# Block products with seven instead of eight multiplications in an attention and expert chain

## The reference, cut to what matters

```python
# 1. attention with decay, 2 x 8 heads, 768 tokens, head_dim 64, in blocks -> x [1536, 512]
# 2. experts
for e in range(4):                       # w1[e] 512 x 1024, w2[e] 1024 x 512
    h = np.maximum(x @ w1[e], 0.0)
    out += p[:, e:e + 1] * (h @ w2[e])
# 3. projection
a = x @ w1                               # 512 x 1024
b = x @ w2
h = a * b @ w3                           # 1024 x 1024
return h @ w_out                         # 1024 x 512
```

## Time and profile before

| | us |
|---|---|
| median of 3 runs | 829.05 (828.93 to 829.12) |
| the profiled execution | 828.76 |
| its span | 826.9 |
| PE busy | 819.8 |
| DVE, ACT, POOL busy | 272.7, 167.3, 153.8 |

### The profile page before, as it was taken

One profiled execution on the slowest core, in us unless ns is written; L12 is line 12 of the kernel. 1 busy time (PEld: TensorE's weight loads), 2 busy tenths in 40 slices (PEclk: granted clock), 3 DMA queues, 4 the chain that ended last, 5 costly groups with the idle time before them and its releaser, 6 DMA issues.

```text
span 826.9 us, 9271 instructions
## 1 busy us (share of the span) xinstructions
PE 819.8 (99%) x3994; PEld 670.5 (81%) x3994; DVE 272.7 (33%) x415; ACT 167.3 (20%) x281; POOL 153.8 (19%) x202
## 2 busy tenths in 40 slices
PE   9999999999999999999999999999999999999998
...
DMA packets 33544, 47.05 MB, mean 57 GB/s; under 512 B 3544, under 2 KB 13280, under 8 KB 33504
## 3 DMA queue, kind: packets, MB, share of 16 engines
...
...
## 4 chain that ended last, share of the span: by engine, by line
PE 97%; DVE 1%; issue 0%; POOL 0%; ACT 0%; POOLq 0%
PE banks L822 48%; PE banks L837 11%; PE banks L838 11%; PE banks L842 11%; PE banks L735 5%; PE banks L891 3%; PE banks L896 3%; PE banks L892 3%; PE banks L747 1%; PE banks L769 1%; PE banks L777 1%; PE banks L793 1%; PE banks L785 0%; DVE probs L599 0%; DVE fin L710 0%
## 5 line engine op out<-in xcount | busy, mean ns | idle before, releaser
L822 PE MATMUL banks<-xh,uph 128*128 128x512 f32 x480 | 189.6, 395 | 0.0
L822 PE MATMUL banks<-xh,upl 128*128 128x512 f32 x480 | 188.7, 393 | 0.0
L822 PE MATMUL banks<-xl,uph 128*128 128x512 f32 x480 | 187.1, 390 | 0.0
L478 ACT ACTIVATE hidh<-hid 128x512 fp32r<-128x512 f32 x120 | 75.9, 632 | 488.9 <-DVE hid L664 422.5
L664 DVE SCALAR_TENSOR_TENSOR hid<-banks,pb 128x512 f32<-128x512 f32 x96 | 66.3, 690 | 294.3 <-PE banks L822 294.3
L837 PE MATMUL banks<-hidh,dnh 128*128 128x512 f32 x384 | 151.1, 394 | 0.0
L838 PE MATMUL banks<-hidh,dnl 128*128 128x512 f32 x384 | 150.8, 393 | 0.0
L447 POOL TENSOR_TENSOR upl<-raw,uph 128x512 fp32r<-128x512 f32 x40 | 52.2, 1304 | 420.5 <-ACT uph L478 420.5
L558 DVE TENSOR_TENSOR hidl<-hid,hidh 128x512 fp32r<-128x512 f32 x120 | 83.5, 696 | 83.7 <-ACT hidh L478 83.7
L822 PEld LDWEIGHTS banks<-xh,upl 128*128 128x128 f32 x480 | 90.1, 188 | 21.5
L822 PEld LDWEIGHTS banks<-xl,uph 128*128 128x128 f32 x480 | 90.2, 188 | 20.9
...
## 6 DMA issues: line engine op xcount, KB each, us to landing
...
```

Source lines behind the costliest of these rows:

```text
L478: return nc.scalar.activation(dst, src, ACT.Copy)
L822: last = mm(bank, x, y, start=kt == 0 and i == 0, stop=kt == KT - 1 and i == 2)
```

## The change

The weights are taken by pairs of hidden tiles: FG = 4 pairs an expert. For token blocks 0 and 1 the product of a pair is seen as a product of 2 x 2 blocks: the weight's A11, A12, A21, A22 (tile by half of the 512 model columns), the tokens' B11, B12, B21, B22 (half of the model columns by token block). Seven block products, each KH = 2 pieces x 3 = 6 matmuls, replace eight: P1 = A11 B11, P2 = A12 B21, P3 = S4 B22, P4 = A22 T4, P5 = S1 T1, P6 = S2 T2, P7 = S3 T3. S and T are sums of blocks: T is made once per stage of tokens (by DVE, from `acc` before the experts and again before the projection), S for each pair (by POOL, `sums`). Token block 2 is multiplied as before (`third`, 12 matmuls a tile: Ua, Ub). One such unit of work is a run w; 16 serve the experts, 8 the projection (w1 and w2 in turn). The banks X, Y, Z are added to by several products, and DVE takes sums out on the way: v1 (by ACT, `snapshot`), u2, u3, c22, c21, c12.

The six hidden tiles of a run (two tiles by three blocks; ring, hh, hl) meet the second weights in the next run: 12 `group`s of 6 matmuls, each complete in one of five banks, and DVE adds each into `acc` (`add_group`), so the experts are summed in SBUF. For the experts the low part of a hidden tile is made by POOL (`hidden_low`), where DVE made it before. In the projection a first run (w1) leaves its six results in `a_tile`, the second (w2) multiplies by them and DVE makes the low parts.

Further: the folded matrix goes to DRAM and comes back a pair at a time like a weight; the attention's results of chunks 0 to 7 go through `acc` (ACT copies, then ACT and POOL split), those of chunks 8 to 11 are split at once as `xc`; the first two weight pairs are split during the fold, and none during the attention; chunk i is loaded to the place of chunk i - 6. The diff, cut to its core (lines taken out are left out, they stand in the functions printed above):

```diff
+                if 1 <= i <= ST:
+                    pool.wait_ge(b_hi, i)
+                    low(xs_l[:, B11:B21 + 1, :, tokens(i - 1)].rearrange("p b k n -> p (b k) n"),
+                        acc[:, :, tokens(i - 1)],
+                        xs_h[:, B11:B21 + 1, :, tokens(i - 1)].rearrange("p b k n -> p (b k) n")).then_inc(b_lo, 1)
+                if ST < i <= NB:
+                    pool.wait_ge(b_hi, i)
+                    low(xs_l[:, B22, :, tokens(i - 1 - ST)], acc[:, KH:KT, tokens(i - 1)],
+                        xs_h[:, B22, :, tokens(i - 1 - ST)]).then_inc(b_lo, 1)
...
+            def a_low(j):
+                s = j % 2
+                pool.wait_ge(wa_hi, j + 1)
+                low(w_l[s][:, A11:A22 + 1, :], up_src(j), w_h[s][:, A11:A22 + 1, :]).then_inc(wa_lo, 1)
+            def sums(j):
+                r = up_src(j)
+                pool.wait_ge(wa_lo, j + 1)
+                tt(r[:, A11, :], r[:, A11, :], r[:, A21, :], ALU.subtract).then_inc(ws_sum, 1)
+                pool.wait_ge(ws_sum, 4 * j + 1)
+                tt(r[:, A21, :], r[:, A21, :], r[:, A22, :], ALU.add).then_inc(ws_sum, 1)
+                pool.wait_ge(ws_sum, 4 * j + 2)
+                tt(r[:, A22, :], r[:, A22, :], r[:, A11, :], ALU.subtract).then_inc(ws_sum, 1)
+                pool.wait_ge(ws_sum, 4 * j + 3)
+                tt(r[:, A12, :], r[:, A12, :], r[:, A22, :], ALU.subtract).then_inc(ws_sum, 1)
...
+            for w in range(NQ):
+                later = 2 <= w + 1
+                if later:
+                    a_low(w + 1)
+                    sums(w + 1)
+                hidden_low(OUTS * w)
+                if later:
+                    s_low(w + 1)
+                hidden_low(OUTS * w + 1)
+                d_low(w)
+                for k in range(2, OUTS):
+                    hidden_low(OUTS * w + k)
...
+            def a_high(j):
+                if j < 2:
+                    act.wait_ge(up_first_ld[j], 16)
+                else:
+                    act.wait_ge(up_ld[j % 2], 16 * (j // 2))
+                    act.wait_ge(piece_done, made(j - 2, "Ub"))
+                copy(w_h[j % 2][:, A11:A22 + 1, :], up_src(j)).then_inc(wa_hi, 1)
+            def s_high(j):
+                act.wait_ge(ws_sum, 4 * (j + 1))
+                copy(w_h[j % 2][:, S3:S2 + 1, :], up_src(j)).then_inc(ws_hi, 1)
...
+                bank = out_bank(i).rearrange("p (a i) -> p a i", a=HP)
+                if i < NB:
+                    copy(acc[:, :, tokens(i)], bank).then_inc(att_left, 1)
+                    act.wait_ge(att_left, i + 1)
+                    if i == 0:
+                        act.wait_ge(fold_done, FT)
+                    if i < ST:
+                        copy(xs_h[:, B11:B21 + 1, :, tokens(i)].rearrange("p b k n -> p (b k) n"),
+                             acc[:, :, tokens(i)]).then_inc(b_hi, 1)
+                    else:
+                        copy(xs_h[:, B22, :, tokens(i - ST)], acc[:, KH:KT, tokens(i)]).then_inc(b_hi, 1)
+                else:
+                    copy(xc_h[:, :, tokens(i - NB)], bank).then_inc(xc_hi, 1)
+                    if i in (8, 9):
+                        t_high(0, i - 8)
+            for k in (2, 3):
+                t_high(0, k)
+            def snapshot(w):
+                act.wait_ge(piece_done, made(w, "P1"))
+                if w > 0:
+                    act.wait_ge(c21_ready, w)
+                copy(v1[:, :], bank_x).then_inc(v1_ready, 1)
+            def hidden_high(n):
+                Q, k = divmod(n, OUTS)
+                c = ORDER[k] // 2
+                act.wait_ge(r_ready, n + 1)
+                if Q > 0:
+                    act.wait_ge(group_done, GR * (Q - 1) + KT * (c + 1))
+                copy(hh[:, ORDER[k], :], ring_at(n)).then_inc(h_hi, 1)
+            for w in range(NQ):
+                later = 2 <= w + 1
+                snapshot(w)
+                if later:
+                    a_high(w + 1)
+                hidden_high(OUTS * w)
+                if later:
+                    s_high(w + 1)
+                hidden_high(OUTS * w + 1)
+                d_high(w)
+                for k in range(2, OUTS):
...
+            def t1_sum(phase):
+                tt(t1[:, :, :], x12, x11, ALU.subtract).then_inc(t_sum, 1)
+            def t2_sum(phase):
+                dve.wait_ge(b_lo, ST if phase == 0 else NB + KH)
+                dve.wait_ge(t_sum, 4 * phase + 1)
+                tt(x11, x22, t1[:, :, :], ALU.subtract).then_inc(t_sum, 1)
+            def t3_sum(phase):
+                tt(x12, x22, x12, ALU.subtract).then_inc(t_sum, 1)
+            def t4_sum(phase):
+                dve.wait_ge(b_lo, ST if phase == 0 else NB + 2 * KH)
+                dve.wait_ge(t_sum, 4 * phase + 2)
+                tt(x21, x21, x11, ALU.subtract).then_inc(t_sum, 1)
+            def t3_low(phase):
+                dve.wait_ge(t_hi, 4 * phase + 3)
+                sub(xs_l[:, T3, :, :], x12, xs_h[:, T3, :, :]).then_inc(t3_lo, 1)
             dve.wait_ge(state_zero, 1)
...
                 if n < NT - 1:
                     scale_q(i + 1)
...
+            def sum_u2(w):
+                dve.wait_ge(piece_done, made(w, "P6"))
+                dve.wait_ge(v1_ready, w + 1)
+                if w > 0:
+                    dve.wait_ge(c12_ready, w)
+                tt(u2[:, :], v1[:, :], bank_y, ALU.add).then_inc(u2_ready, 1)
+            def sum_u3(w):
+                dve.wait_ge(piece_done, made(w, "P7"))
+                if w > 0:
+                    dve.wait_ge(c22_ready, w)
+                tt(u3[:, :], v1[:, :], bank_y, ALU.add).then_inc(u3_ready, 1)
+            def sum_c22(w, dst):
+                dve.wait_ge(piece_done, made(w, "P5"))
+                dve.wait_ge(u3_ready, w + 1)
+                tt(dst, u3[:, :], bank_z, ALU.add).then_inc(c22_ready, 1)
+            def sum_c21(w, dst):
+                dve.wait_ge(piece_done, made(w, "P4"))
+                tt(dst, v1[:, :], bank_y, ALU.add).then_inc(c21_ready, 1)
+            def sum_c12(w, dst):
+                dve.wait_ge(piece_done, made(w, "P3"))
+                dve.wait_ge(u2_ready, w + 1)
+                tt(dst, u2[:, :], bank_z, ALU.add).then_inc(c12_ready, 1)
...
+            def gate(n, src):
+                j = ORDER[n % OUTS]
+                nc.vector.scalar_tensor_tensor(out=ring_at(n), in0=src, scalar=0.0, in1=pb[:, j // 2, :],
+                                               op0=ALU.max, op1=ALU.mult).then_inc(r_ready, 1)
+            def ring_free(n):
+                if n >= OUTS * NQ:
+                    dve.wait_ge(h_lo, n - 1)
+                elif n >= 3:
+                    dve.wait_ge(h_lo, n - 2)
+            def add_group(g):
+                Q, at = divmod(g, GR)
+                dve.wait_ge(group_done, g + 1)
+                if Q < NQ:
+                    c, d = divmod(at, KT)
                     cols = acc[:, d, c * CW:(c + 1) * CW]
...
+            for w in range(NQ):
+                e, q = divmod(w, FG)
+                n = OUTS * w
+                add_groups(w - 1, (0, 1))
+                sum_u2(w)
+                if w == 0:
+                    t3_low(0)
+                add_groups(w - 1, (2, 3, 4, 5))
+                if q == 0:
+                    for c in range(NC):
+                        dve.wait_ge(pb_ld[c], 16 * (e + 1))
+                dve.wait_ge(piece_done, made(w, "P2"))
+                ring_free(n)
+                gate(n, bank_x)
+                add_groups(w - 1, (6, 7))
+                sum_u3(w)
+                ring_free(n + 1)
+                sum_c22(w, ring_at(n + 1))
+                dve.wait_ge(c22_ready, w + 1)
+                gate(n + 1, ring_at(n + 1))
+                add_groups(w - 1, (8, 9, 10, 11))
+                dve.wait_ge(piece_done, made(w, "Ua"))
+                ring_free(n + 2)
+                gate(n + 2, bank_x)
+                ring_free(n + 3)
+                sum_c21(w, ring_at(n + 3))
+                dve.wait_ge(c21_ready, w + 1)
+                gate(n + 3, ring_at(n + 3))
+                ring_free(n + 4)
+                sum_c12(w, ring_at(n + 4))
+                dve.wait_ge(c12_ready, w + 1)
+                gate(n + 4, ring_at(n + 4))
+                dve.wait_ge(piece_done, made(w, "Ub"))
+                ring_free(n + 5)
+                gate(n + 5, bank_y)
...
+            def times(n, src, a):
+                tt(ring_at(n), src, a, ALU.mult).then_inc(r_ready, 1)
+            def hidden_low(n):
+                dve.wait_ge(h_hi, n + 1)
...
+                    sum_c21(w, a_tile[ORDER[3]])
+                    sum_c12(w, a_tile[ORDER[4]])
+                else:
+                    sum_u2(w)
+                    dve.wait_ge(piece_done, made(w, "P2"))
+                    dve.wait_ge(a_copied, 3 * (Q - NQ) + 1)
+                    ring_free(n)
+                    times(n, bank_x, a_tile[ORDER[0]])
+                    sum_u3(w)
+                    ring_free(n + 1)
```

(72 more changed lines are left out.)

907 lines of the change are left out of this document (488 added, 419 removed).

## The result

The changed kernel takes 804.89 us (median of 4 runs, 803.70 to 804.96), the kernel before beside it 829.02: a ratio of 0.971 (95% interval 0.969 to 0.972). The forecast was 800.0, with a range from 788 to 815. The profiled execution took 804.89 with a span of 803.1; before they were 828.76 and 826.9.

The account below looks back on a forecast made before the run. PE was taken as the bound, matmul count times 0.23 us plus the attention. 828.76 - 33.2 + 0.75 + 1.4 + 0.6 + 1.0 + 0.3 = 799.6, forecast 800 us, range 788 to 815.

Parts of the forecast that it names:

- The count: Expert and projection runs: 138 matmuls instead of 144 per run, 3216 wide ones instead of 3360, saving 33.2 us.
- The pace: Remaining matmuls keep the old 230.6 and 229.6 ns; at 227 ns 10 us more saved, equally far above costs 10.
- Rival (a): Clean pace: six matmuls on a bank without switching run like the fold, 227 ns, giving 790 us; chance 0.14.
- Order in the expert stage: Expert runs of 31.8 us without a stall; DVE 15.9, ACT 8.2, POOL 18.2 us hidden beside PE; tightest slack 0.5 us.
- (b): Boundary stalls: DVE is behind with an addition, each of 24 runs loses about 0.5 us, giving 812; chance 0.16.
- (c): POOL becomes the bound in expert runs through hidden low parts and SBUF shared with DVE, giving 845; chance 0.07.
- Attention and first run: Attention net +0.75 us from DVE slip less removed stalls; first run's waits at P2 and P7 +1.4, bounds 0 and 5.
- Into the projection: First projection run: the third block's low part, four DVE pieces behind u2, comes late for Ua: +0.6 us, bounds 0 and 3.
- the 1.8 us: Sign against the prediction: it is wrong if a low part of POOL takes over 1.8 us.
- Second runs of pairs: Projection: the sum freeing bank Y for Ub queues behind hidden_low; 0.35 us stall, four runs +1.0 us, bounds 0 to 3.
- End: The last twelve groups start on a low part that is 0.3 us late: +0.3 us; tail as before.
- the 227 to 234: Sign against the prediction: it is wrong if PE's pace leaves 227 to 234 ns.

Follow-up runs that it names:

- experiment 5: The changed kernel with block product P5 made twice into its bank, 144 matmuls more: 836.31 us, ratio 1.008 to the kernel before.
- experiment 9: The kernel before, each bank getting its three second-weight matmuls in a row (high by high, high by low, low by high): 828.97 or 829.13 us, ratio 1.000.
- experiment 10: The kernel before, one bank at a time in the second-weight product, but with the old matmul order inside a bank: 828.97 or 829.13 us, ratio 1.000.
- experiment 11: The kernel before as a bench: in ten stretches of the expert stage the second-weight product reads other operands, output not the reference: 825.90 us, one execution.
- experiment 12: The kernel before with only SBUF places changed: hidden tiles moved to the front of the late region, acc and fin behind them: 829.30 us, ratio 1.000.
- experiment 6: The changed kernel with sum c21 before hidden_low in second projection runs, and DVE making most low parts between stages while POOL stays off: 796.37 us, ratio 0.960.
- experiment 7: The 796.37 us version with ACT's copy of bank X moved ahead of the high parts of B22 and T4: 793.42 us, ratio 0.957.
- experiment 2: The changed kernel with POOL's low part of S in the projection made as four operations of 128x256 instead of one: 801.96 us, ratio 0.967.
- experiment 4: The changed kernel with POOL, into the projection, waiting until DVE has made the third block's four low parts: 804.54 us, ratio 0.971.
- experiment 1: The changed kernel with DVE's sum c21 ahead of the low part (hidden_low) in second runs of the projection: 801.98 us, ratio 0.967.
- experiment 8: The 793.42 us version with three changes of order: first-run snapshot earlier, u3 and T4's low part before B22's, last-run c21 after hidden_low: 792.66 us, ratio 0.956.

## Why the prediction was right or wrong

**The count** (-33.2) was right: 3216 wide matmuls, and experiment 5 shows their worth, 31.4 us for 144 with the waits that they cover.

**The pace** was mis-sized. I took 230.6 and 229.6 ns; the changed kernel runs at 226.7 throughout, 10.9 us less. Rival (a) had the size (10 us) and not the reason: it put the loss down to streams in which PE reads hidden tiles or changes banks. Experiments 9 and 10 show that the change of bank is not it. Experiment 11 shows that it is the tile that is read, but not because it is a hidden one: the route weights are as slow, and the groups of the changed kernel read hidden tiles at full pace. What it is about the tiles' place stays open (experiment 12). The fold's 227 ns, which I had as one end, was the pace of this kind of stream, and 230.6 belonged to the kernel before.

**Order in the expert stage** was right: no stall from the first groups to the last run of the experts, DVE 16.0 and POOL 18.2 us of 31.28. Rivals (b) and (c) fall. POOL's stretch is 1371 / 1304 = 1.05 on the hidden tiles. Most of DVE's operations there have an input in a bank and do not meet POOL.

**Attention and first run**: +0.75 became +1.3, +1.4 stayed +1.4, and +0.8 came on top: the first groups wait for POOL's low parts. In the first run, which has no groups, the hidden tiles come within 15 us; the low part of the second weights (2.40 us) goes ahead of the third of them, and two took 1.7 us instead of 1.3 beside DVE. Right in kind, each within its bounds.

**Into the projection** is the step that failed: 0.6 us, bounds 0 and 3, became 9.9 (2.8 at P6, 4.6 at Ua, 2.5 of slow clock). I named the right work, the third block's low parts ahead of Ua, and priced it at bare durations, 0.69 each. They took 1.8, and the double-width low part of T3 2.35 instead of the 1.2 it takes without POOL (experiments 6 and 7). Rows that told this were on the table: q scaling took 0.68 alone and 1.57 beside k_dec. I used them in the attention and not here, and as a factor, where they show a wait for the end of an operation. Experiments 2, 4 and 6 show it. P6 waited for POOL's low part of T2, which I had called covered. POOL was held as well, by DVE's double-width sums: its low parts took up to 2.3 us there, over the 1.8 us that the prediction had named as a sign that it is wrong. The Trainium skill (SBUF — State Buffer, Who interferes with whom) states the rule: the port pair that the two share is an exclusive lock, and a VectorE instruction with two SBUF inputs contends for it with a GpSimd instruction that reads SBUF. For VectorE's 2-port modes it adds that whoever issues first has the pair for the whole instruction and the other blocks. The trace agrees, and shows the same for this two-input operation: 2.23 us beside an operation of 2.40, 1.27 beside quarters of it, 0.68 alone. Of the Trainium skill I had cited only GPSIMD Engine Reference, Key points, which says that they contend and not how. The clock's fall was not in the sum at all, since no wait as long was forecast.

**Second runs of pairs**: +1.0, bounds 0 and 3, became +4.5, in three of the four runs. The mechanism was the predicted one, the sum for Ub behind `hidden_low`; the size was off because the 0.68 us were 2.23 there. One edit of order took it away (experiment 1).

**End**: +0.3 became +0.5, beside +0.6 of the same kind ahead of the first projection run, which I had not seen.

So 804.9 instead of 800.0 is two errors against each other: -10.9 that I gave to a rival, and +16 in steps that I had at 4; two of them, priced at 1.6, took 14.4. That the time lay in the range was luck: without the faster pace it would have been 815.8, just outside. The pace of 226.7 ns lies just outside the 227 to 234 that it had allowed. Experiments 6 to 8 won back 12.2 in all.
